# Attention and two gated layers: four chunks of 2, 3, 3 and 4 token tiles instead of three of 4

## What is computed

```python
keep = is_sink | in_window          # 4 sinks, window of 128
a = softmax(where(keep, q @ k.T / sqrt(D), -1e9))
x = (a @ v), as tokens x features   # 1536 x 512
h = x @ w_in                        # 512 -> 2048
x = (h * sigmoid(1.702 * h)) @ w_out
y = (sigmoid(x @ w_gate) * (x @ w_val)) @ w_out2   # 512 -> 1536 -> 512
```

## Time and profile before

| what | value |
|---|---|
| median of 3 runs | 721.55 us (720.5 to 722.55) |
| profiled execution | 719.18 us |
| its span, first to last instruction | 717.4 us |
| PE busy | 687.7 us, 96% |
| DVE, ACT, POOL busy | 56%, 43%, 50% |
| granted clock, mean | 0.997 |
| HBM read and written | 69.57 and 3.15 MB |

### The profile page before, as it was taken

One profiled execution on the slowest core, in us unless ns is written; L12 is line 12 of the kernel. 1 busy time (PEld: TensorE's weight loads), 2 busy tenths in 40 slices (PEclk: granted clock), 3 DMA queues, 4 the chain that ended last, 5 costly groups with the idle time before them and its releaser, 6 DMA issues.

```text
span 717.4 us, 10603 instructions
## 1 busy us (share of the span) xinstructions
PE 687.7 (96%) x3632; PEld 561.6 (78%) x3632; DVE 401.6 (56%) x1032; ACT 310.7 (43%) x643; POOL 361.2 (50%) x419
## 2 busy tenths in 40 slices
PE   6777999999999999999999999999999999999998
PEld 5555788888778877888888778877888888788886
DVE  6888477677666556376776756665343333522222
ACT  4787434445454444354455544444333233322211
POOL 2574345655645644266555655464335446644530
PEclk9999999999999999999999999999999999999999
DMA  6322332344333213143225423311142233323001
GB/s 195 139 74 75 114 117 103 99 138 147 117 118 114 92 60 104 60 147 118 106 100 176 125 82 132 119 59 31 59 146 89 91 126 141 110 89 120 0 1 58
DMA packets 23798, 73.40 MB, mean 102 GB/s; under 512 B 3617, under 2 KB 3617, under 8 KB 23745
## 3 DMA queue, kind: packets, MB, share of 16 engines
q1 hardware_dynamic: 23744, 72.73, 30.0%
HBM read 69.57 MB, written 3.15 MB: 101 GB/s over the span
## 4 chain that ended last, share of the span: by engine, by line
PE 80%; DVE 10%; ACT 5%; issue 3%; SPq 1%; DMA 0%; DVEq 0%; ACTq 0%
PE ps L750 20%; PE ps L751 19%; PE ps L752 19%; PE ps L816 4%; PE ps L817 4%; PE ps L818 4%; DVE g_lo L597 2%; DVE g_hi L595 1%; DVE probs_n L571 1%; DVE gated L588 1%; DVE probs_sink L569 1%; ACT probs L431 1%; PE ps L720 1%; PE ps L707 1%; PE ps L735 1%
## 5 line engine op out<-in xcount | busy, mean ns | idle before, releaser
L376 POOL TENSOR_TENSOR w_lo<-w_raw,w_hi 128x256 fp32r<-128x256 f32 (+1 forms) x336 | 282.6, 873 | 265.5 <-ACT w_hi L425 265.5
L750 PE MATMUL ps<-x_hi,w_hi 128*128 128x512 f32 x480 | 195.3, 407 | 0.3 <-DVE x_lo L581 0.3
L751 PE MATMUL ps<-x_lo,w_hi 128*128 128x512 f32 x480 | 188.1, 392 | 0.0
L752 PE MATMUL ps<-x_hi,w_lo 128*128 128x512 f32 x480 | 187.6, 391 | 0.0
L425 ACT ACTIVATE w_hi<-w_raw 128x1024 fp32r<-128x1024 f32 (+1 forms) x84 | 104.4, 1242 | 146.1 <-PE ps L752 85.5
L588 DVE SCALAR_TENSOR_TENSOR gated<-squashed,ps 128x512 f32<-128x512 f32 x84 | 57.4, 684 | 145.5 <-PE ps L752 83.5
L752 PEld LDWEIGHTS ps<-x_hi,w_lo 128*128 128x128 f32 x480 | 90.2, 188 | 19.9
L750 PEld LDWEIGHTS ps<-x_hi,w_hi 128*128 128x128 f32 x480 | 90.2, 188 | 14.0 <-DVE x_lo L581 0.8
L751 PEld LDWEIGHTS ps<-x_lo,w_hi 128*128 128x128 f32 x480 | 90.6, 189 | 12.9
L431 ACT ACTIVATE probs<-scores,neg_max 128x260 f32<-128x260 f32 x96 | 48.7, 508 | 77.9 <-DVE neg_max L544 77.3
L750 PE MATMUL ps<-g_hi,w_hi 128*128 128x512 f32 x192 | 75.3, 392 | 3.0 <-DVE g_lo L597 3.0
(11 more groups left out here) (73 smaller groups left out, 1020.7 us busy)
## 6 DMA issues: line engine op xcount, KB each, us to landing
w_raw<-in_w SPq DMA_DIRECT2D x36, 768.0 KB, 4.4
w_raw<-in_w SPq DMA_DIRECT2D x48, 512.0 KB, 3.4
q_raw<-in_q_t SPq DMA_DIRECT2D x48, 128.0 KB, 3.5
k_raw<-in_k_t SPq DMA_DIRECT2D x48, 128.0 KB, 3.4
v_raw<-in_v_t SPq DMA_DIRECT2D x12, 256.0 KB, 3.9
out_x<-out_sb SPq DMA_DIRECT2D x12, 256.0 KB, 3.5
v_sink_raw<-in_v_sink SPq DMA_DIRECT2D x2, 160.0 KB, 2.7
k_sink_raw<-in_k_sink SPq DMA_DIRECT2D x4, 8.0 KB, 2.2
```

What stands on the lines that cost most here:

```text
L376: pool.tensor_tensor(w_lo[:, slot, at:at + part], w_raw[:, slot, at:at + part], w_hi[:, slot, at:at + part].bitcast(F32), ALU.subtract).th ...
L750: pe.matmul(ps[:, bank, :], hi, act_hi, start=first, stop=False)
L751: pe.matmul(ps[:, bank, :], hi, act_lo, start=False, stop=False)
L752: return pe.matmul(ps[:, bank, :], lo, act_hi, start=False, stop=last)
```

## The change

There are four chunks, of 2, 3, 3 and 4 tiles (256, 384, 384 and 512 tokens). The early stage has the 16 units of the first two tiles. Beside the first chunk lie 24 units, beside the second 24, beside the third 32, beside the last none. All that belongs to a chunk's tokens has its width now: the moving operands of `hidden`, `gate`, `value` and `down1`, squashed, gated, g_hi, g_lo, the y copies; `down2` has one group of three matmuls for each tile of the chunk. Weights are loaded and split 28 times a chunk as before, so 112 times instead of 84. `placed` puts the slots evenly over the columns streamed in a chunk, with a hole at the step between the layers; parts of a slot lie 512 columns apart. The counts of waits and stores follow (`copied_before`, `stores_before`), and the early weights move to slots 6, 11 and 16 (of 21).

The diff, cut to its core; what is left out puts `units_beside(c)`, `first_unit_beside(c)`, `tokens(c)`, `FIRST_TILE` and the width n in the place of the constants:

```diff
-NCH = B * S // CH
+CHUNK_TILES = (2, 3, 3, 4)
+NCH = len(CHUNK_TILES)
+FIRST_TILE = tuple(sum(CHUNK_TILES[:c]) for c in range(NCH + 1))
...
-CHUNK_UNITS = CH // P * H
+EARLY_UNITS = CHUNK_TILES[0] * H
...
+def columns_in(c):
+    return CHUNK_TILES[c] * P
+
+def quanta_in_step(c, r):
+    own = [columns_in(c)] * KT
+    if r < LAST_UP:
+        return own + own
+    if r == LAST_UP:
+        return own + own + own
+    if r < PER_CHUNK - 1:
+        return own + own + [DM] * CHUNK_TILES[c]
+    return ([columns_in(c + 1)] * KT if c < NCH - 1 else []) + [DM] * CHUNK_TILES[c]
...
-HOLE = 15
+PART = 512
...
+PARTS = 5
...
-def slot_base(n):
-    return 8 * n if n < HOLE else 127 + (n - HOLE) * 59 // 8
+def units_beside(c):
+    return CHUNK_TILES[c + 1] * H if c < NCH - 1 else 0
...
+@lru_cache(None)
+def placed(c):
+    starts = [0]
+    for r in range(PER_CHUNK):
+        for columns in quanta_in_step(c, r):
+            starts.append(starts[-1] + columns)
+    first_end = starts[first_quantum(c, LAST_UP)]
+    second_start = starts[first_quantum(c, LAST_UP) + 2 * KT - 1]
+    second_end = starts[first_quantum(c, PER_CHUNK - 1)]
+    slots = units_beside(c) + W_LAG
+    spacing = (first_end + second_end - second_start - PARTS * PART) // slots
+    before_hole = (first_end - (PARTS - 1) * PART) // spacing + 1
+    parts = {}
+    for n in range(slots):
+        base = n * spacing if n < before_hole else second_start + (n - before_hole) * spacing
+        for off in range(PARTS):
+            at = next(q for q in range(len(starts)) if starts[q] >= base + off * PART)
+            parts.setdefault(at, []).append((off, n))
+    return parts
 
 def parts_at(c, q):
-    if c == NCH - 1:
-        return []
-    return [(off, n) for n in range(CHUNK_UNITS + W_LAG) for off in range(8) if slot_base(n) + off == q]
+    return placed(c).get(q, []) if c < NCH - 1 else []
...
-EARLY_WEIGHTS = (11, 15, 19)
+EARLY_WEIGHTS = (6, 11, 16)
...
-        early = Flow(CHUNK_UNITS, 2, 3, 4, 5, [5, 0], [6, 1], [O_BANK, 2], fillers=2)
+        early = Flow(EARLY_UNITS, 2, 3, 4, 5, [5, 0], [6, 1], [O_BANK, 2], fillers=2)
...
-            for t in range(2, 5):
+            for t in range(2, CHUNK_TILES[0] + 1):
...
-                dve.tensor_copy(g_hi[:, slot, :], gated[:, slot, :]).then_inc(g_hi_done, 1)
+                dve.tensor_copy(g_hi[:, slot, 0:n], gated[:, slot, 0:n]).then_inc(g_hi_done, 1)
...
-                pe.matmul(ps[:, bank, :], hi, act_hi, start=first, stop=False)
-                pe.matmul(ps[:, bank, :], hi, act_lo, start=False, stop=False)
-                return pe.matmul(ps[:, bank, :], lo, act_hi, start=False, stop=last)
+                pe.matmul(to, hi, act_hi, start=first, stop=False)
+                pe.matmul(to, hi, act_lo, start=False, stop=False)
+                return pe.matmul(to, lo, act_hi, start=False, stop=last)
```

More of the change, by code:

```diff
@@ L1 @@
 from contextlib import ExitStack
+from functools import lru_cache
 import numpy as np
@@ L247, in tokens, with width, copied_before, stores_before @@
         def tokens(c):
-            return slice(CH * c, CH * c + CH)
+            return slice(P * FIRST_TILE[c], P * FIRST_TILE[c + 1])
+        def width(step):
+            return columns_in(step // PER_CHUNK)
+        def copied_before(c, parity):
+            return sum((n + 1 - parity) // 2 for n in CHUNK_TILES[:c])
+        def stores_before(c, tt):
+            return sum(n > tt for n in CHUNK_TILES[:c])
         @block.sync
@@ L312, in _ @@
                                     load_v(u // H + 1)
[L313 to L315 removed]
+                for tt in range(CHUNK_TILES[c]):
+                    sp.wait_ge(odd_copied if tt % 2 else even_copied, copied_before(c, tt % 2) + tt // 2 + 1)
+                    first = P * (FIRST_TILE[c] + tt)
+                    sp.dma_start(out[first:first + P, :], out_sb[:, tt, :]).then_inc(stored[tt], 16)
             for tt in range(CH // P):
[L317 removed]
+                sp.wait_ge(stored[tt], 16 * stores_before(NCH, tt))
         @block.gpsimd
@@ L583, in gate @@
             def gate(step):
-                r, slot = step % PER_CHUNK, step % 2
+                r, slot, n = step % PER_CHUNK, step % 2, width(step)
                 dve.wait_ge(squash_done, step + 1)
@@ L797, in down1 @@
                 if m == 0 and r == 0 and c > 0:
-                    pe.wait_ge(even_copied, 2 * c)
-                    pe.wait_ge(odd_copied, 2 * c)
-                last = product(Y_BANKS[m], lambda w: w[:, step % RING, DM + m * P:DM + m * P + P],
-                               g_hi[:, step % 2, :], g_lo[:, step % 2, :], r == 0, r == LAST_UP)
+                    pe.wait_ge(even_copied, copied_before(c, 0))
+                    pe.wait_ge(odd_copied, copied_before(c, 1))
+                n = width(step)
+                last = product(ps[:, Y_BANKS[m], 0:n], lambda w: w[:, step % RING, DM + m * P:DM + m * P + P],
+                               g_hi[:, step % 2, 0:n], g_lo[:, step % 2, 0:n], r == 0, r == LAST_UP)
                 if r == LAST_UP:
```

100 lines of the change are left out of this document (47 added, 53 removed).

## The result

The changed kernel takes 803.19 us (median of 4 runs, 801.07 to 806.79), the kernel before on the same chip 721.02 (4 runs): ratio 1.114, 95% interval 1.111 to 1.118. The forecast was 727.0, range 710 to 742. The direction was right, at a forecast chance of 0.51, hardly more than a toss; the size was missed: the profiled execution's span is 804.8 us, 82 above the 722.8 of the sum (by chance also the distance between the two medians).

What follows compares the result with a forecast made beforehand. A chain of latencies bounds the early stage, TensorE's columns the rest. Span 717.4 - 33.2 + 15.8 + 4.6 + 1.2 + 14 + 3 = 722.8, 724.6 with 1.8 around it, 727.0 us as a median; range 710 to 742.

Steps and rivals of the forecast that it cites:

- forecast chance of 0.51: Whole kernel: chance given to slower, against 0.34 for faster and 0.15 for the same.
- part 3: Products in all chunks: narrower and more of them, 0.117 us for 256 columns and 0.172 for 384; +4.6 us.
- Rival D: Narrow products: weight loads bound them, +69 us, about 796 us in all; chance 0.02.
- The last chunk: Chunk of four tiles: no attention beside it, so it lasts as before.
- VectorE as the engine that PE waits for: New first chunk, main forecast: VectorE limits it and gives back half of the early gain; chance 0.48.
- rival C: Chunks beside attention: GpSimd falls behind too, held up on ports shared with VectorE; 743 us in all, chance 0.15.
- part 4: Chunk boundaries: a fourth wait of PE for g_lo at a last up step, +1.2 us (0 to 3).
- Part 1: Early stage: 16 units instead of 32, 16 slots less at 2.08 us each, -33.2 us.
- a way to be wrong: PE's clock: the prediction is wrong if the granted clock falls where PE pauses; no size given.
- Part 5: Fourth pass over the weights: VectorE's time a step exceeds PE's, +14 us in the first chunk, +3 in a three-tile chunk.
- "fits" by the prediction: Three-tile chunk with 24 units beside it: 0.83 slots a step, so the engines' work fits.
- +3 was given: Three-tile chunk with 32 units beside it: VectorE 5.3 us a step against PE's 5.20, +3 us (0 to 8).

Runs made afterwards that it cites:

- Experiment 15: Kernel before with the transposes at quantum 2 instead of 3 of each slot and pt at 3: 721.98 us, ratio 1.001.
- 7: Changed kernel with four chunks of three tiles and early weights at slots 8, 13, 18: 758.49 us, 1.052 of the kernel before.
- 13: Kernel before with the transposes at quantum 4 instead of 3 of each slot and pt at 5: 745.93 us, ratio 1.033.
- experiment 5: Changed kernel with a PSUM bank of its own for the first chunk's transposes: 791.19 us, 1.099 of the kernel before.
- Experiment 17: Experiment 10 with GpSimd's w_lo pieces cut to an eighth in most steps, so not the full computation: 737.32 us, 1.022 of the kernel before.
- 10: Changed kernel with the edits of experiments 5 and 6 together: 776.54 us, 1.077 of the kernel before.
- experiment 12: Experiment 10 with a unit weighed three slots after its scores instead of two: 781.03 us, 1.082 of the kernel before.
- 6: Changed kernel with transposes at part 2 instead of 3 of a slot and pt at 3 instead of 4, all chunks: 787.79 us, 1.094 of the kernel before.
- experiment 11: Experiments 6 and 7 together, four chunks of three tiles with transposes one part earlier: 747.48 us, 1.036 of the kernel before.
- experiments 13 to 15: Kernel before with the transposes at quantum 4, 5 and 2 instead of 3, pt one after them: 745.93, 768.76 and 721.98 us.

## Why the prediction was right and wrong

**Right.** The products' spacings: 256 columns come 0.12 us apart (65.46 and 65.58 in PE's timeline), 384 columns 0.17 to 0.175, against 0.117 and 0.172 in part 3:

```profile
65.46 0.28 PE L802 MATMUL ps<-g_hi,w_hi 128*128 128x256 f32 x1
65.58 0.28 PE L803 MATMUL ps<-g_lo,w_hi 128*128 128x256 f32 x1
...
240.00 0.33 PE L802 MATMUL ps<-g_hi,w_hi 128*128 128x384 f32 x1
240.17 0.33 PE L803 MATMUL ps<-g_lo,w_hi 128*128 128x384 f32 x1
```

Rival D is out. The last chunk lasts as long as before (188.7 us; before, 528.0 to 717.4, 189.4). Slower was right, and so was VectorE as the engine that PE waits for. GpSimd makes VectorE late, but is no bound: PE's list has no wait for w_lo, so rival C as put is out. The boundaries (part 4) came within their bounds of 0 to 3: of the six waits for g_lo, 6.7 us, four stand at the last up steps and make 4.8 us, +1.8 where 1.2 was given. The other two, 1.9 us, come early in the first and second chunk, beside the attention.

**Part 1, the early stage: -28.8, not -33.2.** The q_hl copies at 18.38, 28.69 and 38.19 us lie 10.3 and 9.5 apart, where the earlier trace rows gave 8.3. The granted clock of the early stretch is 0.85, where the earlier trace rows has 0.98: three falls in 44 us, of 6.8, 3.4 and 3.4 us, where before one lay in 72. The prediction named this as a way to be wrong, and put no number on it. Experiment 15 gives one: its early stage is that of the kernel before, but had six falls of 3.4 us instead of one, and its first squashed came at 91.1 us instead of 85.6, some 1.1 us a fall. Up to the first squashed the changed kernel spent 13.7 us at half clock and the kernel before 3.4; at that rate this is some 3.3 of the 4.4 us missed, an estimate.

**Part 5, the stalls of VectorE: +17 in the sum, some +102 measured** (47, 15 and 40 over PE alone, falls of the clock included). This is the step that failed, and it failed in its form. It compared VectorE's time in a step with PE's, as though work could slide within a step; the parts' positions it took for granted. But the slots' rules were in the change: spacings of 2432, 3697 and 2827 columns, parts 512 apart. The bank that scores and transposes share was in the code. The time from the transposes to pt_lo's end, 2.7 us, was in the timeline of the kernel before. The sum that should have been made is scores times what is missing: 24 x (2.7 - 1.19) = 36 us in the first chunk, 32 x (2.7 - 1.7) = 32 in the third. It would have shown 68 of the 102 us, and it is rough: with the old need of 2.7 it gives nothing for the second chunk and for experiments 7 and 13, which lost 15, 41 and 24 us, because the need moved with the order in VectorE's queue. Of the measured stalls, in the runs:

- first chunk, 47 us: 16 by the shared bank (experiment 5), 16 by the cut of w_lo once the bank is out of the way (17 against 10), some 3 of them by three falls of the clock that went too, and 15 left. The round of VectorE and ScalarE (12) is in these 15; how they split is open.
- second chunk, 15 us, "fits" by the prediction: 2 by the position of the transposes (6), 11 by the cut of w_lo (17), 2 left.
- third chunk, 40 us where +3 was given: 12 by the position (6), 10 by the cut of w_lo (17), 18 left. With the transposes a part earlier its distance is 2.4 us, still short of 2.7; that this is the 18 wasn't tried, since it has no bank to spare.

That VectorE's work and ordered waits would pass PE's time in the first chunk was right, as experiment 12 shows. What failed is the step from there to PE: PE meets VectorE once a slot at a fixed place and stalls there whenever pt_lo is late, and what it loses in one slot doesn't come back in the next.

**The clock.** The prediction had no term for it. Its mean is 0.972, and 0.94 to 0.97 in the four stretches of the first and third chunk, against 1.00 in the chunks of the earlier trace rows. There are 12 falls to half clock where the kernel before had one (and a second in its last 1.2 us). Each of the 12 began during a pause of PE of 2.0 to 2.7 us or within 2 us after it, so they follow the stalls. What they cost can be estimated from runs of one kernel, which differ in their falls. The clock lost in a run is the span times what its mean clock lacks to 1. Of the changed kernel, the run with a mean clock of 0.972 lost 22.5 us of clock and has a span of 804.8 us; that with 0.983 lost 13.6 and has 799.1: 5.7 us for 8.9, 0.64 for one. The 41 runs of the kernel before beside the experiments, clock 0.985 to 0.998, give 0.61 by a fitted line, and the early stages above 0.64. At 0.62 the profiled execution lost some 14 us to the clock where the kernel before lost 1, and by the medians of the runs some 8 of the 82 us are the clock's. It is an estimate, since no run sets the falls. Experiment 17 has one fall in its chunks, and its third chunk is still 18 us above PE alone.

**The rule of the Trainium skill** that the prediction weighed ("SBUF — State Buffer", "SBUF: two separate sides") agrees with the traces for VectorE: its instructions on SBUF are longer beside w_lo, and w_lo cut away gave 27 and 39 us. For GpSimd, which the rule would hold up in turn, they show no price: a w_lo piece of 256 columns takes 0.74 us at the median before and after, GpSimd is busy 57% of the span, and w_lo never ends a wait of PE.

No version tried was faster than the kernel before. The best of those with four chunks that compute everything was experiment 11, 747.48 us.

## What to carry to other kernels

When work in slots is laid beside a stream that gets shorter, first find each place where the slot's own operations take turns on one resource (here a PSUM bank: scores, read, transposes, read), and compare the time needed between two of them, read in the old timeline, with the columns that the new spacing leaves there; multiply what is missing by the number of slots. Then ask what the new order puts ahead of the last reader in its engine's queue, since the need moves with that (2.2 to 3.3 us in experiments 13 to 15, with the same work). Busy shares don't show it: VectorE looked 63% busy and PE idled. The test that settles it is cheap: move the operation within the old kernel's slot, and see at which distance it begins to stall.

## What the runs showed of the hardware

- Two engines in ordered turns can set the pace with neither full: in experiment 12 VectorE was busy 47.5 of 65 us and ScalarE 35.9, VectorE waited 13.5 us for ScalarE and ScalarE 29.1 for VectorE, and PE idled 10.9 us.
- Beside GpSimd's 256-column subtractions VectorE's SBUF-only operations on 256 columns took 0.79, 0.59 and 0.65 us (g_lo, g_hi, probs_n), and 0.52, 0.42 and 0.45 with these cut to an eighth; one that reads PSUM took 0.41 and 0.42.
- The granted clock fell to half for 3.4 us at a time (once 6.8): 12 times in the changed kernel, each in a pause of PE of 2.0 to 2.7 us or within 2 us after it. It had 18 such pauses. The kernel before had four pauses of 1.9 to 2.2 us and one fall ahead of its last 1.2 us. Between runs of one kernel, a us of clock lost went with some 0.6 us of time (an estimate from their spans and mean clocks).
